# Fused attention, gate and spatial MLP on one core: means summed in their own pair, w_val pieces one pair ahead, four fused groups among the val groups

## What is computed

```python
# attention: q, k, v are (2, 8, 768, 64); each query sees 31 near keys and 24 block keys
k_sum = k.reshape(B, H, nb, block, D).max(axis=3)          # max of each block of 32 keys
v_sum = v.reshape(B, H, nb, block, D).mean(axis=3)         # mean of each block of 32 values
scores_l_m = np.where(mask_l, scale * q @ k.T, -1e9)       # |i - j| < 16
scores_s = scale * q @ k_sum.T + np.log(block)
a = softmax(concat(scores_l_m, scores_s));  x = a @ concat(v, v_sum)      # heads side by side: (2, 768, 512)
# gate: a causal convolution of 5 taps for each channel
x = (sigmoid(conv(x, conv_w)) * (x @ w_val)) @ w_out
# spatial MLP
h = np.maximum(x @ w_in, 0.0);  u, v = halves of h
v_n = layernorm(v);  v_s = einsum('ts,bsd->btd', w_spatial, v_n) + b_spatial
out = (u * v_s) @ w_out2
```

## Time and profile before

| what | value |
|---|---|
| median of 3 executions | 309.9 us (309.04 to 312.29) |
| the profiled execution | 309.19 us |
| its span in the profile | 307.5 us |
| PE busy | 292.3 us, 95% of the span |
| DVE busy | 174.0 us, 57% |
| ACT busy | 150.2 us, 49% |
| POOL busy | 123.3 us, 40% |
| granted clock of TensorE | 1.00 |
| moved by DMA | 25.52 MB |

### The profile page before, as it was taken

The page is one execution under the profiler, slowest core; times in us unless marked ns, Lnnn a source line. Parts: engine busy times, 40 slices in busy tenths (PEclk is TensorE's granted clock), DMA queues, the critical chain, the costliest instruction groups (busy, mean ns, idle before and its releaser), DMA issues.

```text
span 307.5 us, 5355 instructions
## 1 busy us (share of the span) xinstructions
PE 292.3 (95%) x1768; PEld 268.6 (87%) x1768; DVE 174.0 (57%) x579; ACT 150.2 (49%) x463; POOL 123.3 (40%) x140
## 2 busy tenths in 40 slices
PE   7779899999799988999999999999999999999996
PEld 6679798999799987788999998888899999988885
DVE  6879899999769899962100006788755242310000
ACT  3669999999976765452222224333332112122221
POOL 6333777879533875550000001343576323220000
DMA  7998999994810623000000001121100000002222
GB/s 161 226 229 180 190 223 210 230 224 100 211 37 0 188 88 102 0 3 0 0 2 0 0 2 51 51 71 51 34 35 2 0 0 2 0 35 88 84 102 102
DMA packets 51801, 25.52 MB, mean 83 GB/s; under 512 B 44586, under 2 KB 46910, under 8 KB 51774
## 3 DMA queue, kind: packets, MB, share of 16 engines
q1 hardware_dynamic: 51774, 25.18, 33.6%
HBM read 22.03 MB, written 3.15 MB: 82 GB/s over the span
## 4 chain that ended last, share of the span: by engine, by line
PE 66%; ACT 7%; DVE 7%; issue 3%; POOL 3%; DMA 2%; SPq 1%; DVEq 0%; ACTq 0%; POOLq 0%
PE psum L691 57%; DVE psum L1048 4%; ACT probs L829 3%; PE psum L636 3%; PE psum L607 2%; PE psum L621 2%; DVE work L1113 1%; PE psum L781 1%; DVE gate L1048 1%; DMA raw<-in_moe_w_out_dram 1%; POOL win_u_lo L516 1%; DMA raw<-in_moe_w_in_dram 1%; ACT qT L817 1%; PE psum L572 1%; ACT probsT L843 1%
## 5 line engine op out<-in xcount | busy, mean ns | idle before, releaser
L516 POOL TENSOR_TENSOR g_lo<-work,g_hi 128x384 fp32r<-128x384 f32 x32 | 32.3, 1023 | 35.9 <-ACT g_hi L955 26.3
L516 POOL TENSOR_TENSOR vn_lo<-work,vn_hi 128x512 fp32r<-128x512 f32 x12 | 15.5, 1293 | 72.9 <-DVE vn_hi L1150 72.9
L829 ACT ACTIVATE probs<-neg_s,neg_max 128x120 f32<-128x120 f32 x96 | 36.7, 387 | 1.2 <-DVE neg_max L974 1.1
L607 PE MATMUL psum<-k_win,qT 128*128 128x120 f32 x192 | 29.0, 274 | 1.7 <-POOL k_win L465 0.9
L636 PE MATMUL psum<-probsT,v_win 120*128 120x128 f32 x192 | 29.9, 278 | 0.0
L974 DVE CUSTOM_DVE_ANT_0 neg_s<-psum,mask 128x120 f32<-128x120 f32 x96 | 24.5, 276 | 4.7 <-PE psum L607 4.6
L607 PEld LDWEIGHTS psum<-k_win,qT 128*128 128x128 f32 x192 | 25.2, 191 | 2.1 <-POOL k_win L465 1.1
L1048 DVE SCALAR_TENSOR_TENSOR psum<-xT,conv_c,psum 128x384 f32<-128x384 f32 x48 | 26.1, 617 | 0.6 <-ACT psum L871 0.4
L636 PEld LDWEIGHTS psum<-probsT,v_win 120*128 120x128 f32 x192 | 25.2, 191 | 0.5
L1128 DVE TENSOR_TENSOR wsp_lo<-psum,wsp_hi 128x384 fp32r<-128x384 f32 x12 | 6.6, 549 | 33.3 <-ACT wsp_hi L936 33.3
L955 ACT ACTIVATE g_hi<-work 128x384 fp32r<-128x384 f32 x16 | 8.3, 523 | 34.8 <-DVE work L1162 34.8
(11 more groups left out here) (125 smaller groups left out, 714.7 us busy)
## 6 DMA issues: line engine op xcount, KB each, us to landing
v_win<-in_v_dram SPq DMA_DIRECT2D x16, 240.0 KB, 3.8
k_nat<-in_k_dram SPq DMA_DIRECT2D x16, 192.0 KB, 4.5
v_nat<-in_v_dram SPq DMA_DIRECT2D x8, 384.0 KB, 5.0
out_dram<-work SPq DMA_DIRECT2D x11, 256.0 KB, 2.0
q_nat<-in_q_dram SPq DMA_DIRECT2D x14, 192.0 KB, 3.8
raw<-in_moe_w_spatial_dram SPq DMA_DIRECT2D x6, 384.0 KB, 3.0
raw<-in_moe_w_out_dram SPq DMA_DIRECT2D x8, 256.0 KB, 2.7
raw<-in_moe_w_in_dram SPq DMA_DIRECT2D x8, 256.0 KB, 3.5
```

The source lines that it names most:

```text
L516: nc.gpsimd.tensor_tensor(dst_lo, src, dst_hi.bitcast(F32), ALU.subtract).then_inc(lo_sem, 1)
L607: ins = nc.tensor.matmul(bank_s(i)[:, g, :], qT[:, s, 2 * t + g, :], k_win[:, s, 2 * t + g, :], start=True, stop=True)
L829: ins = nc.scalar.activation(probs[:, i % RING, g, :], neg_s[:, i % 3, g, :], ACT.Exp, bias=neg_max[:, i % 4, g:g + 1], scale=-1.0, accum_ ...
```

## The change

Five edits:
- **Means in their own pair.** PE's means(p) and ACT's take_means(p) move from t = 5 of pair p - 1 to t = 2 of pair p. POOL's add_v(p) moves from its iteration p - 1 to the start of iteration p. SP no longer loads v_nat(1) ahead of the first v_win; v_nat(p + 1) is issued in iteration p between load_v(p) and the q halves of pair p + 2, where before v_nat(p + 2) stood behind them.
- **w_val one pair ahead.** `WVALS_OF` and `PIECES_OF`: pieces 0 to 3 are loaded in iterations 1 to 4 and split in 2 to 5; pieces 4 and 5 are loaded in 5, 6 in 6, 7 in 7.
- **Four fused groups among the val groups.** `FUSED_AFTER`: fused 0 to 3 stand behind val 5, 7, 9 and 11, in `groups` (PE and the banks) and in `between` (ACT and DVE).
- **The last lower x copy on ACT.** `x_on_dve`: the copy with j = 22 (of 24) goes from DVE's iteration 52 to ACT's. `wait_x` counts accordingly.
- PE's waits before the transposes of the probabilities and POOL's in spread_means follow the new order of the means.

```diff
--- before.py
+++ after.py
@@ -240,13 +240,17 @@
         def bank_x(i):
             return psum[:, 6 + (i // 2) % 2, :].rearrange("p (g n) -> p g n", n=P)
 
+        def x_on_dve(j):
+            return j % 3 == 1 and 2 * j < STEPS - 4
+
         def wait_x(eng, tiles):
 
             n = tiles // 2
             eng.wait_ge(xA_ready, n)
-            eng.wait_ge(xB_ready, n - (n + 1) // 3)
-            if n >= 2:
-                eng.wait_ge(xD_ready, (n + 1) // 3)
+            on_dve = sum(x_on_dve(j) for j in range(n))
+            eng.wait_ge(xB_ready, n - on_dve)
+            if on_dve:
+                eng.wait_ge(xD_ready, on_dve)
 
 
 
@@ -276,8 +280,12 @@
 
 
         BANKS, VALS = (0, 1, 3, 2, 6, 7), 2 * B * C
-        groups = [("val", n) for n in range(VALS)]
-        groups += [("fused", n) for n in range(2 * C)]
+        groups = []
+        for n in range(VALS):
+            groups += [("val", n)]
+            if n in FUSED_AFTER:
+                groups += [("fused", FUSED_AFTER.index(n))]
+        groups += [("fused", n) for n in range(len(FUSED_AFTER), 2 * C)]
         groups += [("u", n) for n in range(2 * B * C)]
         for n in range(B * T):
             groups += [("turned", n), ("v", n)]
@@ -322,7 +330,9 @@
             if c + 1 < C:
                 between += [("win", 2 * c + 2), ("win", 2 * c + 3)]
             between += [("val", 2 * c), ("val", 2 * c + 1)]
-        between += [("fused", n) for n in range(2 * C)]
+            if 2 * c + 1 in FUSED_AFTER:
+                between += [("fused", FUSED_AFTER.index(2 * c + 1))]
+        between += [("fused", n) for n in range(len(FUSED_AFTER), 2 * C)]
 
         LATER = 2 * (TAPS - 1)
 
@@ -401,16 +411,16 @@
             load_heads(1, k_h, k_nat, k_loaded, k_turned)
             load_v_nat(0)
             load_heads(1, q_h, q_nat, q_loaded, q_turned)
-            load_v_nat(1)
             load_v(0)
             for p in range(PAIRS):
                 if p + 2 < PAIRS:
                     load_heads(p + 2, k_h, k_nat, k_loaded, k_turned)
                 if p >= 1:
                     load_v(p)
+                if p + 1 < PAIRS:
+                    load_v_nat(p + 1)
                 if p + 2 < PAIRS:
                     load_heads(p + 2, q_h, q_nat, q_loaded, q_turned)
-                    load_v_nat(p + 2)
                 for n in PIECES_OF[p]:
                     load_piece(n)
             for n in range(PAIRS, len(pieces)):
@@ -492,7 +502,7 @@
                     pool.wait_ge(x_split, p - 1)
                     pool.wait_ge(x_summed, T * (p - 1))
                 else:
-                    pool.wait_ge(v_nat_added, 2 * p + 1)
+                    pool.wait_ge(v_nat_added, p + 1)
                 src = v_mean[NEAR:KEYS, p % 2, :].rearrange("n (a d) -> n a d", a=1).broadcast_to((NB, GROUPS, P))
                 nc.gpsimd.tensor_copy(v_win[NEAR:KEYS, p % 2, :, :], src).then_inc(means_spread, 1)
                 pool.wait_ge(means_spread, p + 1)
@@ -524,17 +534,13 @@
             make_mask()
             make_sel()
             k_tails(0)
-            add_v(0)
             for p in range(PAIRS):
-                if 1 <= p < PAIRS - 1:
-                    add_v(p + 1)
+                add_v(p)
                 if p >= 2:
                     split_x(p - 2)
                 spread_means(p)
                 if p + 1 < PAIRS:
                     k_tails(p + 1)
-                if p == 0:
-                    add_v(1)
                 for n in WVALS_OF[p]:
                     split_wval(n)
             for p in range(PAIRS - 2, PAIRS):
@@ -612,8 +618,8 @@
 
                 if i >= 1:
                     pe.wait_ge(probsT_ready, i)
-                if i % T == 1:
-                    pe.wait_ge(v_mean_ready, min(i // T + 2, PAIRS))
+                if (i + 2) % T == 0 and i + 2 < STEPS:
+                    pe.wait_ge(v_mean_ready, (i + 2) // T + 1)
 
             def turn_probs(i):
                 pe.wait_ge(probs_ready, i + 1)
@@ -741,12 +747,10 @@
                 if i >= STEPS:
                     n, term = divmod(i - STEPS, 3)
                     val(n, (term,))
-                if i == 2:
-                    means(0)
                 if 5 <= i < STEPS + 5:
                     clear_probs(i - 5)
-                if p + 1 < PAIRS and t == T - 1:
-                    means(p + 1)
+                if p < PAIRS and t == 2:
+                    means(p)
                 if 5 <= i < STEPS + 5:
                     turn_probs(i - 5)
                 if 6 <= i:
@@ -848,7 +852,7 @@
                 p, r = divmod(2 * j, T)
                 nc.scalar.activation(by_group(x_of(p, r * P, 2 * P)[0:D]), bank_x(2 * j)[0:D, :, 0:GROUP],
                                      ACT.Copy).then_inc(xA_ready, 1)
-                if j % 3 != 1:
+                if not x_on_dve(j):
                     nc.scalar.activation(by_group(x_of(p, r * P, 2 * P)[D:P]), bank_x(2 * j)[D:P, :, GROUP:P],
                                          ACT.Copy).then_inc(xB_ready, 1)
 
@@ -892,10 +896,8 @@
                 p, t = divmod(i, T)
                 if 5 <= i < STEPS + 5:
                     take_probsT(i - 5)
-                if i == PIECES:
-                    take_means(0)
-                if t == T - 1 and p + 1 < PAIRS:
-                    take_means(p + 1)
+                if p < PAIRS and t == 2:
+                    take_means(p)
                 if p + 1 < PAIRS and t >= PIECES:
                     turned_q(p + 1, t - PIECES)
                 if i < STEPS:
@@ -1090,7 +1092,7 @@
                         max_k(p + 1, t - 1)
                 if i % 2 == 1 and 3 <= i < STEPS + 3:
                     invert_sums((i - 3) // 2)
-                if i >= 8 and i % 6 == 4:
+                if i >= 8 and i % 2 == 0 and x_on_dve((i - 8) // 2):
                     take_x((i - 8) // 2)
                 if p == PAIRS - 1 and t - 1 in WOUT_AT:
                     split_wout(WOUT_AT.index(t - 1))
@@ -1164,8 +1166,9 @@
 
 RING = 6
 VALS_IN = 2
-WVALS_OF = ((), (), (), (0,), (1,), (2,), (3,), ())
-PIECES_OF = ((), (), (0,), (1,), (2,), (3,), (4, 5, 6), (7,))
+FUSED_AFTER = (5, 7, 9, 11)
+WVALS_OF = ((), (), (0,), (1,), (2,), (3,), (), ())
+PIECES_OF = ((), (0,), (1,), (2,), (3,), (4, 5), (6,), (7,))
 WOUT_AT = (0, 1, 3, 4)
 DRAIN_TAPS = (0, 0, 0, 2, 2, 2, 3, 3)
 FIRST_AT = (48, 49, 52, 53)
```

## The result

In 20 executions each, the changed kernel took 308.5 us in the median (308.20 to 308.86) and the kernel before 309.78 (307.94 to 312.29). The ratio is 0.995, with an interval of 0.993 to 0.997: 1.3 us faster, where 4.9 were forecast and 302.4 to 308.2 was the range. Two executions in this document (one of the kernel before on chip 0, 313.03 us, and one of "fused and x", 312.05) fell in a slower state and are left out of the ratios.

The account below looks back on a forecast made before the run. ACT was taken to bound the attention loop and PE alone the kernel from 127.47 us. Gains of 1.1 (attention), 1.2 (w_out) and 2.3 (fused groups) made 4.6, so 304.6 us, set at 305.0; range 302.4 to 308.2.

Parts of the forecast that it names:

- What bounds the kernel: ACT sets the attention loop's pace, DVE and PE are busy in val, PE alone runs from 127.47 us on.
- Means at the start, 1.3 us: At 17.27 us PE's 2.59 us wait for POOL's sum of v_nat(1) goes; 1.3 us gained, k_nat(2) being late next.
- v_nat(2) late, taking 1.0 back: At pair 2's means v_nat(2), issued later, lands after 4.9 to 5.0 us and cuts the head start from 1.3 to 0.3.
- the means hold PE: Rival: v_nat takes 6.3 us, costing 2.4 us together at pairs 2, 5 and 6; time 307.4, chance 0.20.
- slower: Rival: v_nat takes 7.7 us, costing 8.8 us over pairs 2 to 6; time 313.8, chance 0.04.
- the start is kept: Rival: v_nat(2) lands in 3 us, the attention term is 2.4 us; time 303.7, chance 0.14.
- The wait at 37.89, 0.8: PE's 0.92 us wait for POOL's k_tails(3), before the fourth pair's scores, goes; 0.8 us gained.
- Later pairs: I count no loss: In pairs 3 to 6 v_nat would be there with margins of 1.9, 1.3, 0.9 and 0.6 us; no loss.
- The attention term with w_out: Attention loop gain of 1.1 us (bounds -0.6 to 2.8) plus 1.2 for the w_out wait (at worst 0.5).
- w_out, 1.2: PE's 1.22 us wait for the last w_out piece at 83.22 goes; 1.2 us gained, at worst 0.5.
- x on ACT, 1.4: Before val: DVE's first conv taps start 1.5 us earlier relative to PE, ACT's and POOL's work behind them some 1.4.
- Fused groups: In val: PE waits of 0.5, 0.3 and 1.3 us, DVE's cycle 7.6; u starts 2.3 us earlier, bounds 0.5 to 4.1.

Follow-up runs that it names:

- fused and x: The kernel before with only the four fused groups among the val groups and the last lower x copy on ACT; 307.21 us, ratio 0.9937.
- the kernel before with one matmul: The kernel before with one matmul instead of three for the block means of v, leaving out two thirds of the sum; 310.74 us, ratio 1.0020.
- the means put back: The changed kernel with the means, and POOL's and SP's order, back in the sixth step of the pair before; 307.57 us, ratio 0.9925.
- the means-alone kernel: The kernel before with only its means moved to the third step of their own pair; 310.69 us, ratio 1.0004.
- the kernel with wu_lo later: The changed kernel with DVE's low part of the four early fused groups held until after the next gate's taps; 307.00 us, ratio 0.9897.
- the means at t = 1: The changed kernel with the means one step earlier, in the second step of their own pair; 306.90 us, ratio 0.9922.
- the w_val pieces alone: The kernel before with only the w_val pieces and their splits one pair ahead; 309.67 us, ratio 1.0000.
- the fused groups alone: The kernel before with only the four fused groups set among the val groups; 309.43 us, ratio 0.9994.
- the x copy moved: The changed kernel with DVE's attention x copy in the third step and both copies of the fifth on ACT; 309.41 us, ratio 0.9960.

## Why the prediction was wrong

By its own steps:

- *What bounds the kernel*: right. ACT paces the loop, PE the rest, and "what an earlier start gives is kept only if nothing holds ACT up later" is what happened.
- *Means at the start, 1.3 us*: 1.6 (the turn of k_nat(2) began at 17.08, before at 18.70). Right.
- *v_nat(2) late, taking 1.0 back*: wrong. 4.9 us and more was the landing behind the q halves; in the new place in the queue it is 3.6 to 4.6, and PE never waited for v_nat's sum. The two rivals that need a late v_nat (the means hold PE; slower) fall. The first rival, the start is kept, was right in this: pair 3 began 1.99 us early. Its time of 303.7 still failed, by the step after next.
- *The wait at 37.89, 0.8*: gone, but it is gone too in three kernels without this edit (both fused ones, and the kernel before with one matmul). Part of it was chance.
- *"Later pairs: I count no loss"*: this is the step that failed. I checked only whether v_nat would be there in time. I moved 0.65 us of matmuls from a step in which ACT had an x copy to do meanwhile to one in which it had none, and didn't look at ACT's row ahead of the probsT copy. Priced: 0.67 us a pair, of which 0.5 is ACT's idle time and 0.17 its longer busy time. With the last pair's share (19.06 us from its first scores to val 2, against 18.12 with the means put back) it turned a lead of 1.99 us into a lag of 1.11. The attention term with w_out was +2.3; it measured -1.1, below even its lower bounds together (-0.6 + 0.5).
- *w_out, 1.2*: 0.7 in the two kernels that have the w_val pieces and the old means. ACT had idled only 0.51 us there, the price I had named as "at worst". In the changed kernel the lag alone would have left 0.29 of the wait (the means-alone kernel).
- *x on ACT, 1.4*: near; 1.2 us of the val part's gain is this copy (55.80 to 54.57 us).
- *Fused groups*: waits 0.5, 0.3 and 1.3 were forecast, 0.44, 0.28 and 1.14 came; DVE's cycle 7.6 and 7.68. The gain was 1.76, not 2.3. Two of the waits cost 0.17 more each by starts than listed, and the first matmuls after each take 0.1 longer, 0.5 together for these two, as the kernel with wu_lo later shows (1.98 for the listed 1.42).

At full clock the parts compose as follows, each step with its kernel: 309.2 before; 307.0 with fused groups and x; 307.3 with the w_val pieces as well; 308.5 with the means as well. So two parts of the change gain 2.2 us, and the other two take 1.5 back. The second step (0.3) is within its scatter; the third has its mechanism in the rows and in the kernels with the means moved or shortened.

Open: why ACT is busy 0.17 us longer in a pair with the means at t = 2 and why the means at t = 1 still cost 0.2 us a pair, how much of the 37.89 wait the edit itself removes, and what the w_val pieces alone are worth.

## What to carry to other kernels

In this loop, whose pace one engine sets, work on another engine was free, or nearly so, only in the steps where the pacing engine had something of its own in front of the hand-over that this work delays. Before moving it, read the pacing engine's row just ahead of that hand-over in the old step and in the new one; one step further can be worth 3 us in 308. And look for the loss in the pacing engine's own row, as idle time first (0.5 of 0.67 us here): the wait that shows on its partner can sit in another step.

## What the runs showed of the hardware

The prediction took the granted clock as 1.00 throughout, from one execution. It isn't in most others. With the old place of the means PE waits about 2.6 us near 17 us, and in 37 of the 67 executions of the kernel before whose clock is on record the mean was 0.995 or less. In a profile where this happened (the fused groups alone), PE, which had waited 2.55 us for v_nat's sum until 16.79, went to half clock (0.50 is 1.2 GHz) at 18 us and came back by 22:

```profile
17.00:18.00 1.00, 1.00 (x11) 1.00 (x11) 0.40 (x1) 0.04 (x1) 0.00 (x0) 1.00 1.15 203
18.00:19.00 1.00, 0.99 (x6) 0.74 (x5) 0.40 (x3) 0.95 (x4) 0.00 (x0) 0.51 1.25 201
19.00:20.00 1.00, 1.00 (x7) 1.00 (x6) 0.76 (x4) 1.00 (x7) 0.00 (x0) 0.50 0.78 209
20.00:21.00 1.00, 1.00 (x7) 1.00 (x6) 0.07 (x1) 0.82 (x5) 0.00 (x0) 0.50 1.15 319
21.00:22.00 1.00, 1.00 (x9) 1.00 (x9) 0.62 (x6) 0.07 (x1) 0.29 (x1) 0.78 1.32 252
```

The kernel before took 309.22 us in the median at 0.999 or more (30 executions), 310.34 where the mean clock was near 0.994 (26) and 311.88 where it was 0.989 (11). None of the 56 executions of the kernels with the means in their own pair fell below 0.999, if those with the x copy moved are left out; of these ten one did. So the falls became rare with this edit, which took the 2.6 us wait away. But the wait is neither needed nor enough. The profiled execution before had the same 2.59 us and stayed at 1.00. That of the w_val pieces alone had 2.60 us at 17.29 and stayed at 1.00 there; its clock fell at 40 us, behind the wait of 1.86. And that of the kernel with the x copy moved fell at 18 us although its longest wait ahead was 1.01 us, with others close before it (PE busy for 1.79 of 3 us):

```profile
15.00:18.00 3.00, 1.79 (x12) 1.43 (x13) 2.87 (x18) 2.47 (x12) 0.46 (x2) 1.00 1.19 276
18.00:22.00 4.00, 4.00 (x24) 4.00 (x23) 2.78 (x16) 2.27 (x10) 1.00 (x1) 0.57 1.18 198
```

All the falls in these profiles came behind waits of PE; what decides between the same rows with a fall and without one is open.

For the times this means: the means alone, read as "no change" (310.69 against 310.43), are 1.5 us slower than the kernel before at equal clock (309.22), and of the changed kernel's 1.3 us only 0.7 are left there (309.22 to 308.50). The changed kernel's narrow spread, 0.7 us against 4.4, comes with the new place of the means too (0.9 us in the kernel with the means alone), but not through the clock only: the 30 executions before at full clock still lie between 308.00 and 311.07.
